# Attention and two MLPs on one core: values' products of three pairs in one block, and longer lags in the first 14 pair steps

## The reference

```python
def _attn_ref(q, k, v, n_sink, window):         # B=4, H=8, S=768, D=64; n_sink=4, window=128
    scores = scale * np.matmul(q, k.transpose(0, 1, 3, 2))
    is_sink = pos[None, :] < int(n_sink)
    rel = pos[:, None] - pos[None, :]
    keep = is_sink | ((rel >= 0) & (rel < int(window)))
    scores = np.where(keep, scores, -1000000000.0)
    scores = scores - np.max(scores, axis=-1, keepdims=True)
    a = np.exp(scores)
    a = a / (np.sum(a, axis=-1, keepdims=True) + 1e-09)
    return np.matmul(a, v).astype(np.float32)

def _moe_ref(x, w_in, w_out):                   # 3072 tokens, 512 -> 2048 -> 512
    h = x @ w_in
    g = h - np.tanh(h)
    return (g @ w_out).astype(np.float32)

def _moe2_ref(x, modality_id, w_gate, modality_bias, w1, w2):   # 8 experts, 512 -> 1024 -> 512, top 1
    logits = x @ w_gate + modality_bias[modality_id]
    e_idx = np.argmax(logits, axis=1)
    gate_w = softmax(logits)[chosen]
    out[mask] = gate_w[mask, None] * (np.maximum(x[mask] @ w1[e], 0.0) @ w2[e])   # for each expert e

def reference(**kwargs):
    x = attention output as (B*S, H*D)
    return _moe2_ref(_moe_ref(x, ...), ...)
```

## Time and profile before

| | |
|---|---|
| median of 3 runs | 1053.33 us (1053.15 to 1053.75) |
| the profiled execution's own time | 1051.26 us |
| its span in the trace | 1049.7 us |
| TensorE matmuls, busy | 963.0 us (92%), 7646 instructions |
| VectorE, ScalarE, GpSimd, busy | 617.0, 532.2, 454.1 us |
| first stage, up to the first `mlp_in` | 0 to 88.81 us |
| windows with pairs in them | 88.81 to about 670 us |

### The profile page before, as it was taken

How to read it: one execution, slowest core, us unless ns; L and a number is a source line. 1 busy time by engine, 2 the same in 40 slices (tenths; PEclk the granted TensorE clock), 3 DMA queues, 4 the chain that set the end, 5 groups by cost and what they waited for, 6 DMA issues and landing times.

```text
span 1049.7 us, 23285 instructions
## 1 busy us (share of the span) xinstructions
PE 963.0 (92%) x7646; PEld 605.3 (58%) x7646; DVE 617.0 (59%) x1573; ACT 532.2 (51%) x1329; POOL 454.1 (43%) x760
## 2 busy tenths in 40 slices
PE   3447988999999999999999999999899999899996
PEld 2333544565555565565556556555577777677773
DVE  7454876668666757776756765547584334732321
ACT  4445776656656665655665665446422223522221
POOL 5755887735535643545653631210132322222322
PEclk9776999999999999999999999999999999999998
DMA  9503121314411323322122221050215112111111
GB/s 348 190 18 108 47 62 39 101 43 129 102 47 42 90 65 108 86 67 59 42 75 58 73 60 29 2 201 21 28 35 202 51 50 55 31 50 40 50 50 39
DMA packets 50293, 78.51 MB, mean 75 GB/s; under 512 B 14688, under 2 KB 35680, under 8 KB 48672
## 3 DMA queue, kind: packets, MB, share of 16 engines
q1 hardware_dynamic: 41312, 64.01, 20.5%
q0 software_dynamic: 5728, 13.43, 4.2%
q10 hardware_dynamic: 3168, 0.02, 0.2%
HBM read 45.35 MB, written 14.12 MB: 57 GB/s over the span
## 4 chain that ended last, share of the span: by engine, by line
PE 69%; DVE 9%; POOL 8%; issue 6%; ACT 4%; DVEq 1%; DMA 1%; SPq 1%; ACTq 0%; POOLq 0%
PE acc L861 18%; PE h_ps L805 17%; PE h_ps L1986 5%; PE s_ps L1935 5%; PE pt_ps L1935 5%; PE acc L1986 5%; PE x_out L760 3%; PE s_ps L612 3%; PE s_ps L912 2%; PE pt_ps L679 1%; POOL pt L694 1%; POOL v_lo L536 1%; POOL v_raw L518 1%; POOL qk_raw L432 1%; PE x_out L1912 1%
## 5 line engine op out<-in xcount | busy, mean ns | idle before, releaser
L861 PE MATMUL acc<-w_out_all,g_hi 128*128 128x512 f16 x768 | 228.6, 379 | 0.0
L805 PE MATMUL h_ps<-xt_hi,w_in_all 128*128 128x384 f16 x960 | 197.2, 329 | 5.7 <-DVE g_raw L826 4.5
L861 PE MATMUL acc<-w_out_all,g_lo 128*128 128x512 f16 x384 | 146.1, 381 | 2.7 <-DVE g_lo L846 2.7
L805 PEld LDWEIGHTS h_ps<-xt_hi,w_in_all 128*128 128x128 f16 x960 | 92.7, 100 | 60.3 <-issue 3.8
L103 POOL TENSOR_TENSOR tick<-tick 1x1 f32<-1x1 f32 x83 | 16.4, 197 | 251.4 <-ACT y L2002 118.0
L861 PEld LDWEIGHTS acc<-w_out_all,g_hi 128*128 128x128 f16 x768 | 75.1, 98 | 77.8
L817 ACT ACTIVATE g_raw<-h_ps,batch_scale 128x384 f32<-128x384 f32 x120 | 69.5, 579 | 98.6 <-PE h_ps L805 98.6
L846 DVE SCALAR_TENSOR_TENSOR g_lo<-g_raw,batch_scale,g_hi 128x384 f16<-128x384 f32 x128 | 89.7, 701 | 44.6 <-ACT g_hi L836 43.4
L694 POOL TENSOR_SCALAR_AFFINE_SELECT pt<-merged 128x512 f16<-128x512 f16 x96 | 67.6, 704 | 107.3 <-DVE merged L688 107.0
L836 ACT ACTIVATE g_hi<-g_raw,batch_scale 128x384 f16<-128x384 f32 x128 | 79.0, 617 | 45.5 <-DVE g_raw L826 43.3
L805 PE MATMUL h_ps<-xt_lo,w_in_all 128*128 128x384 f16 x480 | 99.0, 330 | 0.0
(11 more groups left out here) (322 smaller groups left out, 2185.0 us busy)
## 6 DMA issues: line engine op xcount, KB each, us to landing
qk_raw<-in_qk SPq DMA_DIRECT2D x31, 454.0 KB, 3.5
raw<-in_w SPq DMA_DIRECT2D x16, 512.0 KB, 7.5
v_raw<-in_v SPq DMA_DIRECT2D x4, 1536.0 KB, 7.3
x_tokens<-x SPq DMA_DIRECT2D x24, 256.0 KB, 3.0
w_in_all<-in_w_in SPq DMA_DIRECT2D x4, 1024.0 KB, 10.0
w_out_all<-in_w_out SPq DMA_DIRECT2D x4, 1024.0 KB, 13.2
kh_stack<-k_hi SPq DMA_DIRECT2D x60, 65.5 KB, 2.1
kl_stack<-k_lo SPq DMA_DIRECT2D x60, 65.5 KB, 2.1
```

Source lines behind the costliest of these rows:

```text
L805: mm = eng.matmul(h_of(m, f), w16[0][:, f, x * DM + k * P:x * DM + (k + 1) * P], r[:, par, k, :], start=(i == 0), stop=(i == 3 * KD - 1))
L861: mm = eng.matmul(acc[t][:, :], l[f % 2][:, t * P:(t + 1) * P], w16[1][:, f, x * DM:(x + 1) * DM], start=(f == 0 and i == 0), stop=(f == N ...
```

## The change

Two things are changed. In `weigh_values` the products of all three pairs of a group are issued in one block where those of the third pair stood, ordered by key block and within it by the three products; nothing is issued any more behind the first and the second pair. `pv_done` now counts groups. The matmuls are the same in number and shape. In the first stage the order of the steps is another: TensorE issues the next pair's scores ahead of the transposition, ScalarE the normalised rows of a pair ahead of the transposed half of the pair before; the sinks' transposition comes last in a step; and the tables place the conversions of groups 2 to 5 and the preparation of the values at other steps.

```diff
@@ weigh_values
         def pv_count(r):
-            return sum(not is_first(i) for i in range(r + 1))
+            return (r + 1) // TPC
...
-                need(eng, q["pv_done"], pv_count(TPC * (g - 2) + (1, 2, 2)[t]))
+                need(eng, q["pv_done"], pv_count(TPC * (g - 1) - 1))
...
-            if E == "pe" and not is_first(r):
+            if E == "pe" and t == TPC - 1:
                 eng.wait_ge(q["parted"], parts(r))
...
+                    for b in range(1 if a % 2 == 0 else 0, TPC + 1):
+                        tiles = slice(max(b - 1, 0), min(b + 1, TPC))
+                        out = x_out[half, tiles.start * P:tiles.stop * P].rearrange("p (b c) -> p b c", c=P)
+                        cols = slice(2 * of_t + max(2 * b - 1, 0), 2 * of_t + min(2 * b + 1, 2 * TPC))
+                        for pt_of, values in ((pt_lo, v_hi), (pt_hi, v_lo), (pt_hi, v_hi)):
+                            yield out, values[par][:, HP * (block_0 + b) + hp, at:at + D], pt_of[:, cols, :]
@@ conversions, prepare_alone
-                early = {1: (None, 0, 1, 2), 2: (4, 5, 6, 7), 3: (8, 9, 10, 11), 4: (13, 14, 15, 16), 5: (19, 20, 21, 22)}
+                early = {1: (None, 0, 1, 2), 2: (2, 3, 5, 6), 3: (8, 9, 12, 13), 4: (14, 15, 18, 19), 5: (19, 20, 23, 24)}
-                if i == tops[2]:
+                if i == tops[2] + (E == "pool" and 2 <= g <= 5):
...
-            for blk in {0: (0,), 1: (1, 2), 2: (3,), 3: (4, 5)}.get(i, ()):
+            for blk in {0: (0,), 1: (1, 2), 4: (3,), 5: (4, 5)}.get(i, ()):
...
-            if i == (4 if E == "dve" else 5):
+            if i == (6 if E == "dve" else 7):
...
-            if i == 8:
+            if i == 9:
@@ alone
-            weighed = {5: (1,), 7: (2,), 8: (4, 5)}
+            weighed = {6: (1,), 7: (2,), 8: (4, 5)}
...
                 if E == "pe":
-                    stage(transpose_probs, E, eng, r - 1)
                     if r + 1 < ALONE:
                         score_pair(E, eng, r + 1)
+                    stage(transpose_probs, E, eng, r - 1)
...
                 if E == "act":
                     score_pair(E, eng, r)
+                    normalise(E, eng, r)
                     stage(transpose_probs, E, eng, r - 1)
-                    normalise(E, eng, r)
```

More of the change, by code:

```diff
@@ L552, in sink_halves @@
                 if b == 0:
-                    eng.wait_ge(q["conv_lo"], 8)
+                    eng.wait_ge(q["conv_lo"], 7)
                 if b:
@@ L727, in weigh_values @@
             par = (a // 2) % 2
-            last = t == TPC - 1
             pt_hi, pt_lo, pt_sinks = pt[:, g % 2, 0:12], pt[:, g % 2, 12:24], pt[:, g % 2, 24:24 + TPC]
-            if E == "pe" and not is_first(r):
+            if E == "pe" and t == TPC - 1:
                 eng.wait_ge(q["parted"], parts(r))
[L732 to L741, removed]
+                eng.wait_ge(q["pt_lo_done"], turned(r) + 2)
+                need(eng, q["xt_lo_done"], g)
+                if a % 2 == 0:
+                    eng.wait_ge(q["v_lo_done"], NB2 * (a // 2) + TPC)
                     eng.wait_ge(q["vs_lo_done"], a // 2 + 1)
+                else:
+                    eng.wait_ge(q["v_lo_done"], NB2 * (a // 2 + 1))
                 block_0 = TPC * (a % 2) - 1
@@ L747, in head_products @@
                     half, at, of_t = slice(D * x, D * (x + 1)), 2 * D * x, TPC * (1 - x)
[L748 to L757, removed]
+                    for b in range(1 if a % 2 == 0 else 0, TPC + 1):
[4 more added lines that the diff above has]
+                            yield out, values[par][:, HP * (block_0 + b) + hp, at:at + D], pt_of[:, cols, :]
                 for i, both in enumerate(zip(head_products(1), head_products(0))):
                     for o, l, x in both:
-                        mm = eng.matmul(o, l, x, start=(begins and i == 0), stop=False, skip_group_check=True)
-                if last:
-                    mm = eng.matmul(x_out.rearrange("p (t c) -> p t c", t=TPC), vs_all[par][:, hp * P:(hp + 1) * P],
-                                    pt_sinks, start=False, stop=True, skip_group_check=True)
-                mm.then_inc(q["pv_done"], 1)
+                        eng.matmul(o, l, x, start=(i == 0), stop=False, skip_group_check=True)
+                eng.matmul(x_out.rearrange("p (t c) -> p t c", t=TPC), vs_all[par][:, hp * P:(hp + 1) * P], pt_sinks,
+                           start=False, stop=True, skip_group_check=True).then_inc(q["pv_done"], 1)
         score_readers = []
@@ L1209, in prepare_alone @@
                 late_constants(E, eng)
-            if i == (3 if E == "dve" else 4) and E in ("dve", "pe"):
+            if i == (5 if E == "dve" else 6) and E in ("dve", "pe"):
                 spread(E, eng, 0)
-            if i == (4 if E == "dve" else 5):
+            if i == (6 if E == "dve" else 7):
                 v_scales(E, eng, 0)
@@ L1327, in alone @@
                     stage(transpose_probs, E, eng, r - 1)
-                for i in (2 * r, 2 * r + 1):
-                    if i:
-                        conversions(E, eng, i)
-                    if i == 2 * r + (E in ("act", "dve")):
-                        stage(transpose_sinks, E, eng, r - 1)
-                    if i == 2 * r:
-                        for of in weighed.get(r, (r - 2,) if r > 8 else ()):
-                            stage(split_x, E, eng, of)
-                    prepare_alone(E, eng, i)
+                if r:
+                    conversions(E, eng, 2 * r)
+                prepare_alone(E, eng, 2 * r)
+                for of in of_step:
+                    stage(split_x, E, eng, of)
+                conversions(E, eng, 2 * r + 1)
+                prepare_alone(E, eng, 2 * r + 1)
+                stage(transpose_sinks, E, eng, r - 1)
         scored = {2 * (r - ALONE): r for r in range(ALONE)}
```

11 lines of the change are left out of this document (8 added, 3 removed).

## The result

The changed kernel takes 1045.97 us (median of 10 runs, 1040.15 to 1048.59) where the kernel before takes 1053.09 (10 runs, 1050.91 to 1055.08). The ratio is 0.9923, 95% interval 0.9908 to 0.9938: 8.1 us faster (6.5 to 9.7), where 3.0 was forecast. The profiled execution took 1042.25 us, with a span of 1040.7 against 1049.7.

A forecast was written before the change was run, and what follows sets the result against it. TensorE's issue and block changes bound it from 173 us, GpSimd's lateness mattered from 98, a chain bound the first stage; +1.7 + 0.5 − 5.2 = −3.0 us, 1053.33 to 1050.3 us, range 1045 to 1055.5.

The forecast's parts named there:

- The price of a block: Windows from 173 us: entering and leaving a block costs 0.22 us whatever its length; 36 blocks fewer give −7.9 us.
- the gate between 98 and 173 us: Groups 4 to 7: products done before a group's last parting on GpSimd move behind it, +0.48 us in group 5.
- the schedule carried through the first stage: First stage: instructions keep their durations from before through the engines' new orders; first mlp_in at 90.5 us, +1.7.
- The five waits: From 173 us, TensorE's waits ahead of the sinks' transposition (L713) lengthen by 0.54 us each, +2.7 us.
- The window from 98 to 173 us: Groups 4 to 7: saved blocks against products moved behind GpSimd's last partings, sum +0.5 us, bounds −1.8 and +2.
- the forecast's terms for groups 5 to 7: Window from 98 to 173 us: +0.48 us for group 5, −0.06 for group 6, +0.48 for group 7.
- rival E: First slots: a denser end of the first stage brings full clock earlier, −3 us, time 1047; chance 0.10.
- group 4's −0.44: Window from 98 to 173 us: group 4 loses two blocks, its wait not at the third pair, −0.44 us.
- The first stage, +1.7: First stage up to the first mlp_in: 88.81 + 1.1 + 0.6 = 90.5 us, so +1.7 us.
- the end's longer block: End of the first stage: the group's one block has 18 products instead of 12 at half clock, 0.64 us.
- the sum of +1.1: End of the first stage: the sinks' transposition, begun at 83.32 us before, comes 1.1 us later.
- rival B: First stage gains as the longer lag removes waits: first mlp_in at 86 to 87 us, time about 1046; chance 0.20.

The follow-up runs named there:

- e3: Changed kernel with each group's block in the windows cut in three, same matmuls, two more blocks in 28 groups; ratio 1.0026 to the kernel before.
- e4: Changed kernel with v_split of batches 1 to 3 one slot later, so merged stands ahead of v_hi on ScalarE; ratio 0.9874 to the kernel before.
- e1: Kernel before with only the merged blocks of the values' products, first stage and tables as before; ratio 0.9953 to the kernel before.
- e2: Kernel before with only the changed first stage (new order and tables), a block per pair as before; ratio 0.9978 to the kernel before.
- e9: Kernel before with the new tables only, steps in the order of before, a block per pair; ratio 0.9916 to the kernel before.
- e6: Changed kernel with a block per pair kept for groups 0 to 3, merged from group 4 on; ratio 0.9914 to the kernel before.
- e14: e9 with ScalarE taking a pair's normalised rows ahead of the transposed half of the pair before; first mlp_in at 84.84 us.
- e8: Kernel before with the new step order but the old tables, a block per pair; ratio 1.0056 to the kernel before.
- e13: e9 with TensorE issuing the next scores ahead of the transposition; first mlp_in at 84.57 us.
- e16: New tables, steps in the order of before, merged blocks and e10's later split; 1034.36 us, ratio 0.9841 to the kernel before.
- e12: The changed kernel, unaltered, measured and profiled a second time; ratio 0.9920 to the kernel before.
- e10: Changed kernel with e4's later v_split only from window 1 on, window 0 as in the changed kernel; ratio 0.9863 to the kernel before.
- e15: e9 with the sinks' transposition last in its step on each engine; first mlp_in at 82.12 us.

## Why the prediction was right and wrong

Of the 6.0 us by which the changed kernel's trace is below the forecast of −3.0, slots 0 to 16 hold 3.0 (−2.54 instead of +0.5), the first stage 2.0 (−0.27 instead of +1.7), the windows behind them 0.5 and the rest 0.5. The block's price was right. The two steps that failed are the gate between 98 and 173 us and the schedule carried through the first stage; 1.4 us of the 3.0 are the clock's and chance.

**The price of a block: right.** 0.22 us from four block ends; e3 gives 0.20. By the slots it is 3.76 − 3.33 = 0.43 for a group in an odd chunk (1.04 + 1.19 + 1.53 before, twice 0.65 and 2.03 now) and 0.21 in an even one, 12 x 0.64 = 7.7 us against the forecast's 7.9.

**The five waits: right, somewhat small.** L713 went from 2.6 to 6.0 us, +3.4 where 2.7 stood. e4 shows the cause (`v_hi` ahead of `merged`) by taking it away. With 7.7 saved, 3.4 given back and 1.4 less waiting for ScalarE's `normed` (2.2 to 0.8 us), the sum is −5.7, which the trace has; forecast −5.2.

**The window from 98 to 173 us: wrong.** "What was done before the gate is now done behind it" took GpSimd's partings as fixed in time. They are not: GpSimd's queue hangs on what the other engines give it. The transposition ahead of group 5's last partings began 2.02 us earlier, and the last parting 2.03. Towards group 7 GpSimd works without a gap from its wait for ScalarE's half of a weight on, which ended 2.82 us earlier; what moved ScalarE's half was not followed further. Before:

```profile
118.53 0.38 PE L679 MATMUL pt_ps<-ident,normed 128*128 128x128 f32 x2
```
```profile
153.90 0.69 POOL L365 TENSOR_SCALAR w_out_all<-w_out_all,w_scale 128x512 f32<-128x512 f32 x1 [2.36 <-ACT w_out_all L358]
```

Changed:

```profile
116.51 0.38 PE L679 MATMUL pt_ps<-ident,normed 128*128 128x128 f32 x2
```
```profile
151.08 0.69 POOL L365 TENSOR_SCALAR w_out_all<-w_out_all,w_scale 128x512 f32<-128x512 f32 x1 [1.45 <-ACT w_out_all L358]
```

The last partings of groups 5 and 7 and the blocks behind them in the changed kernel:

```profile
123.63 0.63 POOL L697 TENSOR_SCALAR_AFFINE_SELECT pt<-merged 128x512 f16<-128x512 f16 x1
...
168.48 0.95 POOL L697 TENSOR_SCALAR_AFFINE_SELECT pt<-merged 128x512 f16<-128x512 f16 x1
```
```profile
124.32 0.25 PE L751 MATMUL x_out<-pt,v_hi 128*64 128x128 f16 x2 [1.79 <-POOL pt L697]
...
169.50 0.25 PE L751 MATMUL x_out<-pt,v_hi 128*64 128x128 f16 x2 [1.94 <-POOL pt L697]
```

The waits are there as forecast, but the gates opened 2.03 and 2.81 us earlier than in the earlier trace rows, more than the 1.69 by which the stretch began earlier (slot 4). Slots 4 to 16 gave −1.12 in the changed kernel, −1.10 in e1 and 0.0 in e2, instead of about +0.9 of the forecast's terms for groups 5 to 7. In the six profiles with the stretch of half clock (e4, above) this gain is gone again.

**The clock: rival E, half its size, and chance.** Slots 0 to 4 were 1.42 us shorter (1.94 in the second profile), where E took 3; it counted up to five slots at half clock, and before the clock was full in the second (8.7 us behind the first `mlp_in`). Merging has no part in it: with the early rise these slots are 1.44 us shorter in e1 (merged) and 1.51 in e9 (a block per pair), with the late rise 0.05 longer in e6 (merged) and 0.07 in e2 (a block per pair). So group 4's −0.44 of the forecast is not there either. But e3, with the first stage of the changed kernel, has the late rise, e14 and e8, with blocks per pair, have it late, e9 and e13 early, and e16, merged, late. No order of the program that was tried decides it. It goes with the spread of single runs: of the changed kernel's ten, which span 8 us, the two fastest and the profiled one have a mean clock of 0.977 or 0.979 and the three slowest 0.969. The median of these means is 0.974, as in the runs of the kernel before that stand beside e12, so I do not count it to the change's effect.

**The first stage, +1.7: wrong in sum, and two large terms were not seen.** At pairs 3 and 6 the carried schedule held: 24.55 for the exponentials of pair 3 (forecast 24.8), 37.82 for pair 6 (38.1), and the end's longer block cost what it should (e1: +1.13 at pair 13, +1.78 at the first `mlp_in`, so 0.65 against 0.64). Pair 6 was partly luck: e10 has the same first stage and its pair 6 at 36.43 (see the last section). At pairs 10 and 12 the schedule was about 2 us too late: 64.47 (66.4) and 77.90 (80.0):

```profile
24.55 0.35 ACT L635 ACTIVATE probs<-s_ps,neg_max 128x132 f32<-128x132 f32 x1
...
37.82 0.36 ACT L635 ACTIVATE probs<-s_ps,neg_max 128x132 f32<-128x132 f32 x1
...
64.47 0.36 ACT L635 ACTIVATE probs<-s_ps,neg_max 128x132 f32<-128x132 f32 x1
...
77.90 0.35 ACT L635 ACTIVATE probs<-s_ps,neg_max 128x132 f32<-128x132 f32 x1
```

The step that failed is that I carried "each instruction with its duration from before" through the new orders: durations belong to their neighbours. VectorE's L361 in the step of pair 9 took 1.40 us before, where GpSimd's `k_lo` had begun ahead of it, and 0.74 here, where it began ahead of GpSimd's parting (which then took 1.08 us instead of 0.63); and TensorE's clock was full there (0.5 before, 53.2 to 56.6 us). These are two instances; how the whole 2 us are made up is not shown. Before:

```profile
55.85 1.40 DVE L361 SCALAR_TENSOR_TENSOR w_in_all<-w_in_all,w_scale 128x512 f16<-128x512 f32 x1
```
```profile
55.52 1.18 POOL L453 TENSOR_TENSOR k_lo<-qk_raw,k_hi 128x524 f16<-128x524 f32 x1
```

Changed:

```profile
53.98 0.74 DVE L361 SCALAR_TENSOR_TENSOR w_in_all<-w_in_all,w_scale 128x512 f16<-128x512 f32 x1
```

And what the sum of +1.1 (order and tables) hid are the tables' −6.5 (e9) and the order's +4.5 (e13 +2.2, e14 +2.5, e15 −0.2; one profile each). In the changed kernel the longer block then takes its 0.6 back, and the rest is the spread of the first stage. I had weighed rival B by "the longer lag takes waits out of its chain"; the tables' lags do, the steps' new order does the opposite. A sum of both could not show this: it is small because two large terms of opposite sign nearly cancel in it.

## What to carry to other kernels

Where TensorE bounds, count its changes between kinds of matmul: merging two blocks of these products saved 0.2 us each time, whatever their length, and it is tested by cutting a block up, not only by merging. Take a change that touches both an order and a table of places apart before believing either: here one half cost most of what the other gained, and the best kernel keeps only one. A gate that another engine holds is not fixed in time if that engine waits for yours; and before a difference in a stage that one profile shows is explained, the same program's stage in a second profile says how much is chance.

## What the hardware showed that I had not expected

VectorE's smallest instructions wait out GpSimd's. The row sums (L645, two elements a partition) took 0.22 us in e2 and 0.23 in e10, but 1.14 in the changed kernel, of the same pair, beside the same GpSimd work. In order e2, e10 and, twice, the changed kernel:

```profile
34.91 0.22 DVE L645 TENSOR_SCALAR row_sum<-row_sum 128x2 f32<-128x2 f32 x1 [0.90 <-ACT probs L635]
```
```profile
34.94 0.23 DVE L645 TENSOR_SCALAR row_sum<-row_sum 128x2 f32<-128x2 f32 x1 [0.90 <-ACT probs L635]
```
```profile
35.58 1.14 DVE L645 TENSOR_SCALAR row_sum<-row_sum 128x2 f32<-128x2 f32 x1 [0.90 <-ACT probs L635]
```
```profile
34.42 3.38 POOL L536 TENSOR_TENSOR v_lo<-v_raw,v_hi 128x512 f16<-128x512 f32 x3
```

GpSimd's three instructions take 1.13 us each and end near 35.55, 36.68 and 37.80; the row sums began at 35.58, just behind an end, and were done at 36.72, just behind the next. In e2 they began at 34.91, shortly before the end of GpSimd's first (35.08), and were done at 35.13. The Trainium skill, SBUF — State Buffer, section "SBUF: two separate sides", says that the two engines share a port pair that one holds for a whole instruction; the rows agree, for instructions of this form. L361's 1.40 us above fits as well: it ended 0.55 us behind the end of GpSimd's `k_lo` at 56.70.

This is also how a small difference grows. e10 and the changed kernel are the same program up to the first `mlp_in`. Their traces part at 29.3 us, where TensorE transposes the sinks, in the changed kernel and in e10:

```profile
29.33 0.87 PE L713 MATMUL pt_ps<-ident,sinks 128*128 128x128 f32 x3 [0.25 <-DVE merged L688]
```
```profile
29.36 0.52 PE L713 MATMUL pt_ps<-ident,sinks 128*128 128x128 f32 x3 [0.25 <-DVE merged L688]
```

The granted clock is 1.00 from 27 to 32 us in both, so the cause of the 0.35 us stays open. The row sums then begin 0.64 us apart and are done 1.55 us apart, the exponentials of pair 6 come at 37.82 and 36.43, and the first `mlp_in` at 88.54 and 87.06. No run here took the contention away, so what it costs in the whole first stage is not shown; at this one place it is the 0.9 us between 1.14 and 0.23.
